# First tile's attention on f32 operands as loaded, head orders replanned, last sums sent from where their parts were

## The chip, the cores and the metric

The kernel runs on one core of a Trainium2 chip. A core has five engines that each work through their own list of instructions in order and meet at semaphores: TensorE (PE, matrix products into PSUM), VectorE (DVE), ScalarE (ACT), GpSimd (POOL) and SyncE (SP), which here issues every DMA. The metric is the device time of one execution in microseconds; lower is better.

## What is computed

Windowed attention over 32 heads, then two feed-forward blocks over 2304 tokens of width 512:

```python
batch, n_heads, seq, head_dim = (4, 8, 576, 64); window = 64
scores = (1/sqrt(D)) * q @ k.T
mask   = (rel >= 0) & (rel < window)          # rel = query position - key position
attn   = softmax(where(mask, scores, -1e9))
x      = attn @ v                             # then (B*S, H*D) = 2304 x 512
h      = max(x @ w1, x @ w2, x @ w3)          # 512 -> 768
y      = h @ moe_w_out                        # 768 -> 512
h2     = y @ w_in                             # 512 -> 2048
g      = where(h2 >= 1, h2, where(h2 <= -1, 0, (h2 + 1)**2 / 4))
out    = g @ w_out                            # 2048 -> 512
```

Everything is float32 at the input and the output.

## The kernel before

**High and low parts.** Most products are made in three passes on a reduced type (`F32R`). An operand `x` is split: `hi` is a copy into the reduced type, `lo` is `x - hi`. A product is then hi*lo + lo*hi + hi*hi. So every operand costs a copy (`hi`, mostly on ACT) and a subtraction (`lo`, on DVE or POOL). In `order` listings and the profile these copies and subtractions appear under the helper lines L649 (ACT), L875 (DVE) and L1084 (POOL).

**Tiles.** The 2304 tokens are nine tiles of 256, taken in six pieces `PIECES = (1, 1, 1, 2, 2, 2)`. For each tile, attention runs in four steps, one for each pair of heads; there are 36 steps, numbered `s`. The first piece is steps 0 to 3. A step is a chain: load `k`, `q`, `v`; split them (`k_hi`, `q_hi`, `v_hi`, `k_lo`, `q_lo`, `v_lo`); `score` on PE (L523, L525: one matmul of 256 columns and one of 128 for each of four blocks of keys); `mask` (L897) and `max` (L904) on DVE; `exp` (L676) and `safe` (L685) on ACT; `invert` (L911) on DVE; `norm` (L1119) on POOL; `probs`, a transpose on PE (L535); `p_hi` on ACT and `p_lo` on DVE; `values` on PE (L544, L546); `cross` on ACT (L695) and `x_sum` on DVE (L922), which add the two halves of the result; and `x_hi`, `x_lo`, the operands of layer 1.

**Zeros.** The two heads of a pair lie on different partitions, so `qT` holds each head's queries beside zeros. `zeros` on DVE (L942) writes eight blocks of 64x512 before anything else.

**Layer 1.** For each piece, 18 groups of 12 matmuls (L560) multiply `xT` with `w1`, `w2`, `w3` (six groups for each). `group` on ACT or DVE takes the result out of PSUM. The weights come in 12 pieces `w0` to `w11` of 128x768 and are split as well (`w_hi`, `w_lo`); the first six groups need pieces 0 to 3. Group 0 needs `x_lo` of steps 0 to 3.

**Order.** Nothing is scheduled when the kernel runs. For steps up to about the middle of the second piece, the table `FIRST` lists for each engine, word by word, what comes next. After it, `in_order` sorts the rest by planned positions: `SPREAD` and `LAG` say how far `score` and `probs` lie ahead of `values`, in units of a layer 1 group, and `AROUND` where each engine's part of a step lies. `Q_LO_ON_DVE` and `V_HI_ON_POOL` choose the engine of two kinds. An engine never skips an instruction that waits.

**After layer 1.** Layer 2 (L585) and then layers 3 and 4 (L612, L632) follow, PE bound. Layer 4's sums for 384 tokens stay in six PSUM banks over a unit of work; there are six units. The first two leave as partial sums to DRAM (`part_dram`), come back into `part_in` and are added by `block_out` on DVE (L1038): `o_sb[b % 3] = acc4[b] + part_in[b]`. `o_sb` has room for three of the six blocks, so the fourth block waits until the first has been sent: `dve.wait_ge(out_dma[b % QB], 16 * (2 * nth + b // QB))`. After the last block its DMA ends the program.

Of the kernel before, what the change touches and what calls it, by code (L numbers as in the profile page):

```python
# [97 lines left out]
def steps_of(n):  # L98
# [13 lines left out]
        k0 q0 mask0 v0 k1 q1 v1 k2 q2 k3 q3 v2 v3 w0 w1 w2 w3 k4 q4 w4 w5 w6 k5 q5 w7 v4 mask1 w8 k6 q6 w9  # L112
        w10 w11 v5 k7 q7 v6 k8 q8 v7 k9 q9 v8
    """,
    "PE": """
        score0 score1 score2 probs0 values0 score3 probs1 probs2 values1 values2 probs3 values3 score4
        score5 score6 group0 probs4 group1 group2 values4 group3 score7 group4 probs5 group5 group6
        values5 group7 group8 probs6 group9 group10
    """,
    "ACT": """  # L120
        k_hi0 q_hi0 v_hi0 k_hi1 q_hi1 v_hi1 k_hi2 q_hi2 exp0 safe0 k_hi3 q_hi3 exp1 safe1 p_hi0 w_hi0 exp2
        w_hi1 cross0 safe2 v_hi2 q_hi4 p_hi1 x_hi0 k_hi4 w_hi3 p_hi2 exp3 cross1 safe3 q_hi5 v_hi3 x_hi1
        k_hi5 w_hi4 cross2 p_hi3 w_hi7 x_hi2 cross3 q_hi6 k_hi6 exp4 x_hi3 safe4 w_hi11 v_hi5 k_hi7 q_hi7
# [4 lines left out]
        zeros0 zeros1 q_lo0 q_lo1 mask0 max0 q_lo2 invert0 mask1 max1 invert1 mask2 p_lo0 max2 w_lo1
        invert2 x_sum0 mask3 p_lo1 max3 w_lo3 p_lo2 x_sum1 invert3 x_sum2 p_lo3 w_lo7 mask4 x_sum3 max4
        q_lo6 mask5 invert4 max5 q_lo7 mask6 invert5 max6 p_lo4 w_lo5 w_lo9 invert6 w_lo4 w_lo6 x_sum4  # L130
        mask7 p_lo5 max7 group6 invert7 x_sum5 group7 w_lo10 group8 p_lo6 group9
# [1137 lines left out]
```

## Time and profile before

| | us |
|---|---|
| median of three runs | 804.43 (803.88 to 804.71) |
| the profiled execution, its own time | 805.22 |
| span of its trace, first to last instruction | 803.1 |
| PE busy in the span | 773.7 (96%) |
| DVE, ACT, POOL busy | 421.0, 406.5, 437.3 |

The span is what the views show; the execution's own time is 2.1 us longer. Times inside the trace are microseconds from the span's start. A matmul's duration includes its pipeline, so the distance between two starts is the better measure of what one costs. The page's second part gives PE's granted clock in 40 slices: with full speed as 1.0 it is 0.9 and 0.6 in the first two, 0.7 in the third and 1.0 after that apart from one slice at 0.9.

### The profile page before, as it was taken

The numbers are of one execution on the slowest core, as the hardware profiler recorded it, in microseconds if no ns is written. First come the engines' busy times: TensorE is split into PE (matmuls) and PEld (weight loads), VectorE is DVE, ScalarE is ACT, GpSimd is POOL, SyncE is SP. The second block draws the span as 40 slices with busy tenths as digits, with TensorE's granted clock in tenths as the row PEclk, the third lists the DMA queues.
The fourth block names the chain that finished last, engine by engine and source line by source line (L and its number), as shares of the span: only waits on it lengthen the run. The fifth ranks groups of instructions, "written<-read, shape, count | busy, mean of one in ns | idle before, by whom it ended". The sixth has DMA issues, their size and how long they took to land.

```text
span 803.1 us, 12567 instructions
## 1 busy us (share of the span) xinstructions
PE 773.7 (96%) x4320; PEld 704.7 (88%) x4320; DVE 421.0 (52%) x903; ACT 406.5 (51%) x957; POOL 437.3 (54%) x355
## 2 busy tenths in 40 slices
PE   4589999999999999999999999999999999999997
PEld 4589999988888888899997898899888999988996
DVE  6666476544644521227316573374777456357434
ACT  7865788657566322044525455355455446345331
POOL 6867779755666325025517475266666447248221
PEclk9679999999999999999999999999999999999999
DMA  7611322221220021002001102002111001200302
GB/s 233 222 57 57 110 70 81 96 69 55 80 72 27 27 80 52 1 8 98 0 0 52 53 1 79 1 2 80 53 52 53 1 1 61 98 1 27 131 1 79
DMA packets 25193, 46.56 MB, mean 58 GB/s; under 512 B 2352, under 2 KB 5552, under 8 KB 25136
## 3 DMA queue, kind: packets, MB, share of 16 engines
q1 hardware_dynamic: 25136, 45.82, 17.3%
q8 instruction: 33, 0.54, 0.3%
q14 instruction: 24, 0.20, 0.1%
HBM read 37.95 MB, written 7.86 MB: 57 GB/s over the span
## 4 chain that ended last, share of the span: by engine, by line
PE 90%; DVE 5%; ACT 3%; issue 1%; DMA 1%; SPq 0%; DVEq 0%; ACTq 0%
PE wide L560 28%; PE wide L632 22%; PE bank L612 21%; PE wide L585 9%; PE wide L544 3%; PE wide L523 3%; PE bank L535 2%; DVE g_sq L1026 2%; PE wide L546 1%; PE wide L525 1%; ACT g_sq L807 1%; ACT prob L676 1%; DMA v_nat<-v_dram 1%; DVE g L1031 0%; DVE prob L904 0%
## 5 line engine op out<-in xcount | busy, mean ns | idle before, releaser
L560 PE MATMUL wide<-xT,w 128*128 128x256 f32 (+1 forms) x1296 | 241.6, 342 | 0.0
L560 PEld LDWEIGHTS wide<-xT,w 128*128 128x128 f32 x1296 | 200.6, 191 | 23.7
L632 PE MATMUL wide<-w4s,gT 128*128 128x512 f32 x864 | 210.1, 392 | 0.0
L1084 POOL TENSOR_TENSOR gT<-g,gT 128x384 fp32r<-128x384 f32 x96 | 105.6, 1110 | 185.8 <-ACT gT L649 185.8
L612 PE MATMUL bank<-yT,w3s 128*128 128x384 f32 x1008 | 188.9, 337 | 3.1 <-issue 1.6
L632 PEld LDWEIGHTS wide<-w4s,gT 128*128 128x128 f32 x864 | 161.1, 188 | 31.2
L612 PEld LDWEIGHTS bank<-yT,w3s 128*128 128x128 f32 x1008 | 177.8, 188 | 11.2 <-DVE g L1031 4.0
L807 ACT ACTIVATE g_sq<-g_sq,half 128x384 f32<-128x384 f32 x96 | 58.1, 615 | 128.4 <-DVE g_sq L1026 128.1
L1014 DVE TENSOR_TENSOR pu<-bank,pu 128x384 f32<-128x384 f32 x72 | 40.1, 558 | 135.8 <-PE bank L612 129.0
L1031 DVE TENSOR_TENSOR g<-pu,g_sq 128x384 f32<-128x384 f32 x72 | 61.5, 854 | 36.2 <-ACT g_sq L807 35.6
L933 DVE TENSOR_TENSOR h<-wide,h 128x256 f32<-128x256 f32 (+1 forms) x72 | 40.1, 556 | 75.7 <-PE wide L560 75.3
L676 ACT ACTIVATE prob<-prob,neg_max 128x128 f32<-128x128 f32 x144 | 56.0, 391 | 41.9 <-DVE neg_max L904 41.6
L585 PE MATMUL wide<-h1s,wo 128*128 x432 | 75.3, 334 | 0.2 <-DVE h1s L875 0.2
L585 PEld LDWEIGHTS wide<-h1s,wo 128*128 128x128 f32 x432 | 74.9, 188 | 0.5 <-issue 0.5
L1119 POOL TENSOR_TENSOR prob<-prob,row_inv 128x512 f32<-128x512 f32 x36 | 38.1, 1060 | 57.3 <-DVE row_inv L911 57.1
L649 ACT ACTIVATE gT<-g 128x384 fp32r<-128x384 f32 x96 | 47.9, 521 | 41.0 <-DVE g L1031 40.9
L1084 POOL TENSOR_TENSOR v_part<-v_nat,v_part 128x512 fp32r<-128x512 f32 x36 | 47.6, 1322 | 17.9 <-ACT v_part L649 17.6
L1026 DVE TENSOR_SCALAR g_sq<-pu 128x384 f32<-128x384 f32 x72 | 54.0, 751 | 2.5
L523 PE MATMUL wide<-kT,qT 128*128 128x256 f32 x144 | 41.2, 362 | 13.9 <-DVE qT L875 8.5
L803 ACT ACTIVATE pu<-bank 128x384 f32<-128x384 f32 x72 | 34.4, 477 | 23.9 <-PE bank L612 23.9
L544 PE MATMUL wide<-pT,v_part 128*128 128x256 f32 x144 | 38.6, 345 | 7.6 <-DVE pT L875 3.8
L922 DVE TENSOR_TENSOR x_sums<-wide,o_cross 64x256 f32<-64x256 f32 x72 | 30.3, 420 | 29.5 <-ACT o_cross L695 28.4
(69 smaller groups left out, 963.4 us busy)
## 6 DMA issues: line engine op xcount, KB each, us to landing
v_nat<-v_dram SPq DMA_DIRECT2D x36, 256.0 KB, 2.7
raw<-w_dram SPq DMA_DIRECT2D x16, 512.0 KB, 3.5
h<-moe_w_dram SPq DMA_DIRECT2D x12, 384.0 KB, 6.1
out_dram<-o_sb SPq DMA_DIRECT2D x18, 256.0 KB, 2.1
k_in<-k_dram SPq DMA_DIRECT2D x12, 288.0 KB, 3.5
q_in<-q_dram SPq DMA_DIRECT2D x12, 256.0 KB, 2.9
part_dram<-o_sb SPq DMA_DIRECT2D x12, 256.0 KB, 2.1
part_in<-part_dram SPq DMA_DIRECT2D x2, 1536.0 KB, 7.3
```

Source lines behind the costliest of these rows:

```text
L523: pe.matmul(s_ps[:, b, :, :].rearrange("p x n -> p (x n)"), qT[:, n % 2, 0, j, :, :].rearrange("p h n -> p (h n)"), kT[:, n % 2, :, keys], ...
L544: pe.matmul(o_ps[:, b, :, :].rearrange("p x n -> p (x n)"), v_part[:, 0, s % 2, b, :], pT[:, :, s % 2, cols], start=True, stop=False, skip ...
L560: mm = pe.matmul(acc[gr % 2][:, 0:cols], w123[:, wp, w, kc, c * P:(c + 1) * P], xT[:, x_side(t), xp, kc, 0:cols], start=(kc == x == 0), st ...
L585: mm = pe.matmul(acc[c % 2][:, 0:MTOK], wo1[:, wp, kc, c * P:(c + 1) * P], h1s[:, of(t, 1), hp, kc, :].rearrange("p a n -> p (a n)"), star ...
L612: mm = pe.matmul(bank[:, 0:MTOK], w3s[j % HALF_F][:, wp, W_OF[m], kc * P:(kc + 1) * P], yT[:, m, yp, kc, :], start=(m in (0, 1, 3) and kc ...
L632: mm = pe.matmul(acc4[b], gT[:, k, gp, tb * P:(tb + 1) * P], w4s[pair_f(g) % HALF_F][:, wp, f, :], start=(first and x == 0), stop=(last an ...
L649: return act.activation(dst, src, ACT.Copy)
L676: act.activation(prob[:, s % 2, b, :], prob[:, s % 2, b, :], ACT.Exp, bias=neg_max[:, s % 2, b:b + 1], scale=-1.0, accum_out=row_sum[:, s ...
L807: act.activation(g_sq[:, k % 2, :], g_sq[:, k % 2, :], ACT.Square, bias=half[:, 0:1], scale=0.5).then_inc(squared, 1)
L1026: dve.tensor_scalar(g_sq[:, k % 2, :], output(g_at, k), -1.0, 1.0, ALU.max, ALU.min).then_inc(clamped, 1)
L1031: dve.tensor_tensor(g[:, k % 2, :], output(g_at, k), g_sq[:, k % 2, :], ALU.max).then_inc(g_done, 1)
L1084: return pool.tensor_tensor(dst, src, high.bitcast(F32), ALU.subtract)
```

## The change

**First piece plain.** Steps 0 to 3 no longer split `q`, `k`, `v` and the probabilities. `q`, `k` and `v` are loaded straight into their own f32 tiles (`q_plain`, `k_plain`, `v_plain`, one set for each pair), the score and values products are f32 matmuls of 128 columns, `max` reads the mask itself and there is no `mask` step, and the result goes from PSUM to `x_hi` (two halves on ACT) and `x_lo` (two halves, now on DVE) with no `cross` and no `x_sum`. `p_hi` of these steps is a plain copy, and has no `p_lo`. `q_plain` is loaded in two DMAs for each pair, in runs of 64 floats. The zeros of `qT`, which later pieces need, are written by two POOL memsets of 128x2048; DVE writes eight of 64x256 in `q_plain`.

**Orders.** `FIRST`, `SPREAD`, `LAG`, `AROUND`, `Q_LO_ON_DVE` and `V_HI_ON_POOL` have new contents.

**Last sums.** `block_out` on DVE writes its sum over `part_in[b]` instead of into `o_sb`, and SP sends it from there; the wait on `out_dma` is gone. The last block is added and sent in two halves. The reload of `part_in` now waits for the sends of the unit before it.

```diff
 def in_order(engine):
+            if i < PAIRS and (kind in SPLIT_KINDS or (engine, kind) == ("POOL", "x_lo")):
+                continue
...
-SPREAD = {1: (1.43, 2.27), 2: (2.24, 1.07), 3: (0, 2.0), 4: (0.6, 2.1), 5: (0, 1.9)}
-LAG = {1: (5.95, 1.63), 2: (5.04, 1.51), 3: (4.4, 2.1), 4: (5.0, 1.8), 5: (5.3, 1.8)}
+SPREAD = {1: (3.96, 1.1), 2: (3.63, 1.15), 3: (0.52, 1.88), 4: (2.16, 2.13), 5: (1.14, 2.82)}
+LAG = {1: (4.0, 1.44), 2: (4.45, 1.66), 3: (3.67, 1.4), 4: (4.26, 1.96), 5: (5.24, 1.92)}
...
         def k_in_of(n):
+            if a == 0:
+                sp.dma_start(k_plain[n][:, :], k_dram[:, u, start:start + cols]).then_inc(k_plain_in[n], 16)
+                return
...
         def q_in_of(n):
+            if a == 0:
+                for h in range(2):
+                    rows, _ = diagonal(h)
+                    sp.dma_start(q_plain[n][rows, :, h, :],
+                                 q_dram[rows, u, start:start + cols].rearrange("p (j n) -> p j n", n=BLK)).then_inc(q_plain_in[n], 16)
+                return
...
         def come_back(pair):
             for tb in range(QB):
-                sp.wait_ge(out_dma[tb], 16 * 2 * (pair + 1))
+                sp.wait_ge(out_dma[tb], 16 * 2 * (pair + 1 if pair == 1 else len(LEAVE) - 1))
...
+        def plain_score(s):
+            pe.wait_ge(off_diagonal, 2 * (s + 1))
+            pe.wait_ge(q_plain_in[s], 2 * 16)
+            pe.wait_ge(k_plain_in[s], 16)
+            after(pe, mask_added, NB * (scores_before(s) + 1))
+            for b in range(NB):
+                mm = pe.matmul(scores_of(s)[:, b, 0, :], q_plain[s][:, b, :, :].rearrange("p h n -> p (h n)"),
+                               k_plain[s][:, b * BLK:b * BLK + SPAN], start=True, stop=True, skip_group_check=True)
...
+        def plain_values(s):
+            pe.wait_ge(v_plain_in[s], 16)
+            pe.wait_ge(p_hi, s + 1)
+            after(pe, x_plain_lo, 2 * s)
+            for b in range(NB):
+                mm = pe.matmul(o_ps[:, b, 0, :], v_plain[:, s, b, :], p_plain[:, s % 2, b * P:(b + 1) * P],
+                               start=True, stop=True, skip_group_check=True)
...
+        def x_lo_of(s):
+            for h in range(2):
+                rows, cols = diagonal(h)
+                dve.wait_ge(x_plain_hi, 2 * s + h + 1)
+                lo(x_of(s, 1)[rows, :].rearrange("p (b n) -> p b n", b=NB), o_ps[rows, :, 0, cols],
+                   x_of(s, 0)[rows, :].rearrange("p (b n) -> p b n", b=NB)).then_inc(x_plain_lo, 1)
...
-            dve.wait_ge(out_dma[b % QB], 16 * (2 * nth + b // QB))
-            dve.tensor_tensor(o_sb[:, b % QB, :], acc4[b], part_in[:, b, :], ALU.add).then_inc(dve_out, 1)
+            cols = DM // 2 if unit == len(UNIT_PAIR) - 1 and b == BLOCKS - 1 else DM
+            for at in range(0, DM, cols):
+                dve.tensor_tensor(part_in[:, b, at:at + cols], acc4[b][:, at:at + cols], part_in[:, b, at:at + cols], ALU.add)\
+                    .then_inc(dve_out, 1)
...
+        for side in range(2):
+            pool.memset(qT[:, side, :, :, :, :].bitcast(F32), 0.0).then_inc(off_diagonal_parts, 1)
```

How the order moves, at three places. First ACT from its start; `prob` is the exponentials, `pT` and `p_plain` the turned probabilities, `w_50` the weights, `kT`, `qT`, `v_part` the split operands. Before:

```order
2 L649 ACTIVATE kT<-k_in 128x320
3 L649 ACTIVATE qT<-q_in 64x4x64 x2
4 L649 ACTIVATE v_part<-v_nat 128x512
5 L649 ACTIVATE kT<-k_in 128x320
6 L649 ACTIVATE qT<-q_in 64x4x64 x2
7 L649 ACTIVATE v_part<-v_nat 128x512
8 L649 ACTIVATE kT<-k_in 128x320
9 L649 ACTIVATE qT<-q_in 64x4x64 x2
10 L676 ACTIVATE prob,row_sum<-prob,neg_max 128x128 x4
```

And now:

```order
2 L738 ACTIVATE prob,row_sum<-prob,neg_max 128x128 x4
3 L747 ACTIVATE safe<-row_sum,tiny 128x4
4 L738 ACTIVATE prob,row_sum<-prob,neg_max 128x128 x4
5 L747 ACTIVATE safe<-row_sum,tiny 128x4
6 L709 ACTIVATE p_plain<-bank 128x512
7 L738 ACTIVATE prob,row_sum<-prob,neg_max 128x128 x4
8 L709 ACTIVATE w_50<-h_49 128x768
9 L747 ACTIVATE safe<-row_sum,tiny 128x4
10 L709 ACTIVATE xT<-wide 64x256 x2
```

The eight copies of `k`, `q` and `v` that stood ahead of the first exponentials are gone. The second place is PE just before layer 1's first group (L560 before, L616 now). Before, the last matmuls of the score of step 6 stand ahead of it, behind those of steps 4 and 5:

```order
90 L523 MATMUL wide<-kT,qT 128x256
91 L525 MATMUL wide<-kT,qT 128x128
92 L560 MATMUL wide<-xT,w_50 128x256 x12
93 L535 MATMUL bank<-ident,prob 128x128 x4
94 L560 MATMUL wide<-xT,w_50 128x256 x24
```

Now, from the transpose of step 2 on, with the score of step 4 ending at row 20 and that of step 5 beginning at row 22:

```order
9 L578 MATMUL bank<-ident,prob 128x128 x4
10 L586 MATMUL wide<-p_plain,v_plain 128x128 x4
11 L578 MATMUL bank<-ident,prob 128x128 x4
12 L586 MATMUL wide<-p_plain,v_plain 128x128 x4
...
20 L565 MATMUL wide<-kT,qT 128x128
21 L616 MATMUL wide<-xT,w_50 128x256 x36
22 L563 MATMUL wide<-kT,qT 128x256
```

One score (step 4) stands ahead of group 0 instead of three, and the scores of steps 5 and 6 stand behind groups 2 and 5. The third place is SP's first loads; `h_49` is where the weights arrive. Before:

```order
7 L436 DMA v_nat<-v_dram 128x512
8 L424 DMA k_in<-k_dram 128x320
9 L431 DMA q_in<-q_dram 128x256
10 L424 DMA k_in<-k_dram 128x320
11 L431 DMA q_in<-q_dram 128x256
12 L436 DMA v_nat<-v_dram 128x512 x2
13 L446 DMA h_49<-moe_w_dram 128x768 x4
```

And now:

```order
7 L440 DMA k_plain_66<-k_dram 128x320
8 L451 DMA q_plain_62<-q_dram 64x4x64 x2
9 L462 DMA v_plain<-v_dram 128x512
10 L440 DMA k_plain_67<-k_dram 128x320
11 L451 DMA q_plain_63<-q_dram 64x4x64 x2
12 L462 DMA v_plain<-v_dram 128x512 x2
13 L474 DMA h_49<-moe_w_dram 128x768 x8
```

None of the rows up to 13 waits for a buffer any more, each `q` is two DMAs, and eight pieces of weights follow in a row instead of four.

## Rows read from the trace of the kernel before

**Rows 1.** The chain of work that ended last, by engine (the page's fourth part)

```profile
PE 90%; DVE 5%; ACT 3%; issue 1%; DMA 1%; SPq 0%; DVEq 0%; ACTq 0%
```

**Rows 2.** Stretches: from:to, length, busy us of PE, PEld, DVE, ACT, POOL, PEclk, DMA

```profile
10.00:20.00 10.00, 6.97 (x31) 6.26 (x31) 6.02 (x32) 8.74 (x33) 8.23 (x9) 1.00 0.89 295
...
0.00:44.30 44.30, 23.17 (x104) 21.07 (x105) 29.63 (x92) 34.74 (x102) 32.21 (x40) 0.78 0.63 207
44.30:81.00 36.70, 36.70 (x295) 36.70 (x295) 24.49 (x67) 20.41 (x62) 25.02 (x24) 0.93 0.21 62
```

**Rows 3.** Timeline of PE: start, us, what xcount [idle before it <-releaser]

```profile
14.41 1.09 PE L535 MATMUL bank<-ident,prob 128*128 128x128 f32 x4
...
42.56 0.55 PE L523 MATMUL wide<-kT,qT 128*128 128x256 f32 x1 [2.06 <-DVE neg_max L904]
...
44.30 2.87 PE L560 MATMUL wide<-xT,w 128*128 128x256 f32 x12
...
47.67 3.73 PE L560 MATMUL wide<-xT,w 128*128 128x256 f32 x24
...
52.12 1.64 PE L560 MATMUL wide<-xT,w 128*128 128x256 f32 x12
53.59 0.28 PE L523 MATMUL wide<-kT,qT 128*128 128x256 f32 x1
...
54.47 1.65 PE L560 MATMUL wide<-xT,w 128*128 128x256 f32 x12
```

**Rows 4.** Timeline of ACT in the head

```profile
3.07 0.47 ACT L649 ACTIVATE kT<-k_in 128x320 fp32r<-128x320 f32 x1 [0.99 <-DMA k_in<-k_dram]
...
10.89 0.40 ACT L676 ACTIVATE prob<-prob,neg_max 128x128 f32<-128x128 f32 x1 [0.53 <-DVE neg_max L904]
...
13.20 0.84 ACT L649 ACTIVATE qT<-q_in 64x256 fp32r<-64x256 f32 x2
14.24 0.40 ACT L676 ACTIVATE prob<-prob,neg_max 128x128 f32<-128x128 f32 x1 [0.20 <-DVE neg_max L904]
...
15.92 0.30 ACT L685 ACTIVATE safe<-row_sum,tiny 128x4 f32<-128x4 f32 x1
...
16.64 0.84 ACT L649 ACTIVATE w<-h 128x768 fp32r<-128x768 f32 x1
```

**Rows 5.** Timeline of DVE in the head

```profile
10.56 0.29 DVE L904 CUSTOM_DVE_ANT_0 prob<-wide,prob 128x128 f32<-128x128 f32 x1 [0.19 <-DVE prob L897]
...
24.37 1.64 DVE L875 TENSOR_TENSOR w<-h,w 128x768 fp32r<-128x768 f32 x1
```

**Rows 6.** Timeline of POOL in the head

```profile
0.73 0.20 POOL L1130 MEMSET ident<- 128x128 f32 x1 [0.29 <-POOLq L1264]
...
13.23 1.04 POOL L1119 TENSOR_TENSOR prob<-prob,row_inv 128x512 f32<-128x512 f32 x1 [1.61 <-DVE row_inv L911]
...
17.65 1.83 POOL L1084 TENSOR_TENSOR w<-h,w 128x768 fp32r<-128x768 f32 x1
```

**Rows 7.** SP's timeline in the head

```profile
1.65 0.42 SPq L442 DMA_DIRECT2D mask<-masks_dram  x1
```

**Rows 8.** DMA issues of the first 60 us: count, size, median us to landing

```profile
q_in<-q_dram SPq DMA_DIRECT2D x10, 128.0 KB, 3.1
mask<-masks_dram SPq DMA_DIRECT2D x1, 256.0 KB, 4.0
```

**Rows 9.** Timeline around step 8: the last score matmul and the normalization

```profile
78.97 0.22 PE L525 MATMUL wide<-kT,qT 128*128 128x128 f32 x1
...
83.20 1.04 POOL L1119 TENSOR_TENSOR prob<-prob,row_inv 128x512 f32<-128x512 f32 x1 [2.11 <-DVE row_inv L911]
```

**Rows 10.** Timeline of the program's end, all engines

```profile
790.53 8.36 PE L632 MATMUL wide<-w4s,gT 128*128 128x512 f32 x36
...
795.59 2.05 DVE L1038 TENSOR_TENSOR o_sb<-wide,part_in 128x512 f32<-128x512 f32 x3 [3.06 <-PE wide L632]
...
798.50 2.02 DVE L1038 TENSOR_TENSOR o_sb<-wide,part_in 128x512 f32<-128x512 f32 x3 [0.86 <-DMA out_dram<-o_sb]
```

More of the change, by code:

```diff
@@ L118 @@
-        values5 group7 group8 probs6 group9 group10
+        score0 score1 score2 probs0 values0 probs1 score3 values1 probs2 values2 probs3 values3 score4
+        group0 group1 group2 score5 group3 group4 probs4 group5 score6 group6 values4 group7 probs5 score7
+        group8 group9 values5 probs6 group10
     """,
     "ACT": """
-        k_hi0 q_hi0 v_hi0 k_hi1 q_hi1 v_hi1 k_hi2 q_hi2 exp0 safe0 k_hi3 q_hi3 exp1 safe1 p_hi0 w_hi0 exp2
-        w_hi1 cross0 safe2 v_hi2 q_hi4 p_hi1 x_hi0 k_hi4 w_hi3 p_hi2 exp3 cross1 safe3 q_hi5 v_hi3 x_hi1
@@ L123 @@
-        k_hi5 w_hi4 cross2 p_hi3 w_hi7 x_hi2 cross3 q_hi6 k_hi6 exp4 x_hi3 safe4 w_hi11 v_hi5 k_hi7 q_hi7
-        exp5 w_hi9 safe5 p_hi4 group0 exp6 group1 safe6 group2 cross4 v_hi6 w_hi10 group3 k_hi8 group4
-        p_hi5 x_hi4 group5 exp7 safe7 cross5 v_hi7 x_hi5 k_hi9 p_hi6 q_hi8 q_hi9
+        exp0 safe0 exp1 safe1 p_hi0 exp2 w_hi0 safe2 x_hi0 p_hi1 w_hi2 w_hi3 exp3 x_hi1 safe3 p_hi2 w_hi4
+        w_hi7 k_hi4 q_hi4 x_hi2 p_hi3 q_hi5 k_hi5 w_hi9 x_hi3 w_hi10 exp4 group0 safe4 v_hi4 q_hi6 group1
@@ L126 @@
+        k_hi6 group2 k_hi7 q_hi7 w_hi6 group3 v_hi5 group4 p_hi4 exp5 group5 safe5 exp6 cross4 safe6 v_hi6
+        p_hi5 x_hi4 exp7 cross5
     """,
     "DVE": """
[L128 to L131, printed above, removed]
+        zeros0 zeros1 zeros2 zeros3 max0 max1 invert0 invert1 max2 w_lo1 invert2 x_lo0 max3 w_lo3 x_lo1
@@ L132 @@
+        invert3 w_lo7 x_lo2 w_lo5 mask4 x_lo3 max4 w_lo10 invert4 q_lo6 mask5 q_lo7 max5 p_lo4 mask6
+        invert5 max6 group6 w_lo8 invert6 group7 p_lo5 x_sum4 mask7 group8 max7 group9 w_lo11
     """,
     "POOL": """
-        k_lo0 v_lo0 k_lo1 v_lo1 k_lo2 norm0 k_lo3 norm1 w_lo0 w_hi2 norm2 v_lo2 x_lo0 k_lo4 norm3 x_lo1
-        v_lo3 k_lo5 x_lo2 v_hi4 w_lo2 k_lo6 x_lo3 norm4 v_lo4 k_lo7 w_hi5 norm5 w_hi6 norm6 v_lo5 x_lo4
-        v_lo6 w_hi8 norm7 w_lo8 w_lo11
+        norm0 norm1 w_hi1 w_lo0 norm2 w_lo2 norm3 w_hi5 k_lo4 w_lo4 k_lo5 v_lo4 norm4 k_lo6 w_lo6 k_lo7
@@ L137 @@
+        w_hi8 norm5 w_hi11 v_lo5 norm6 w_lo9 x_lo4
     """,
@@ L532, in probs @@
             pe.wait_ge(normed, s + 1)
-            after(pe, p_lo, s - 1)
+            if s < 2 + PAIRS:
+                after(pe, p_hi, s - 1)
+            else:
+                pe.wait_ge(p_lo, s - 1 - PAIRS)
             for b in range(NB):
@@ L565, in _ @@
         for kind, i in in_order("PE"):
-            if kind == "score":
+            if kind == "score" and i < PAIRS:
+                plain_score(i)
+            elif kind == "values" and i < PAIRS:
+                plain_values(i)
+            elif kind == "score":
                 score(i)
@@ L938, in _ @@
             if kind == "zeros":
[L939 to L942 removed]
+                for h in range(2):
+                    rows, _ = diagonal(h)
+                    dve.memset(q_plain[i][rows, :, 1 - h, :], 0.0).then_inc(off_diagonal, 1)
             elif kind == "q_lo":
@@ L954, in _ @@
                 x_sum_of(i)
+            elif kind == "x_lo":
+                x_lo_of(i)
             elif kind == "w_lo":
```

176 lines of the change are left out of this document (104 added, 72 removed).

## The prediction

> **What bounds the kernel now.** I read the chain of waits first: PE carries 90% of it [rows 1]. Nearly all matmuls are untouched by the change, so time can only come from where PE isn't working, from PE's half rate, or from the tail. The windows show where PE isn't working: up to 44.30, where layer 1 begins, PE is busy for 23.17 of 44.30 us; in the 36.70 us after that it never stops [rows 2]. The reader is to see that from 44.30 on the time is a row of matmuls, and that before it ACT is the fullest engine (34.74 us, against 32.21 on POOL and 29.63 on DVE). So the main question is at what time group 0 of layer 1 begins, and the second is what is left for PE then. The last stretch is the end: PE's final matmuls run from 790.53 to 798.89, but DVE's last three sums begin only at 798.50, after 0.86 us of waiting for the send of the first, and end at 800.52; the program ends at 803.1 [rows 10].
>
> **When group 0 begins, worked forward.** Prices first. A score or values step at PE's half rate takes 44.30 - 42.56 = 1.74 us, at full rate 54.47 - 53.59 = 0.88 [rows 3]. Four exponentials take 15.92 - 14.24 = 1.68, `safe` and `p_hi` together 16.64 - 15.92 = 0.72, a weight's `hi` 0.84, `k_hi` 0.47, a two-half copy of 64x256 0.84 [rows 4]; this last is also my price of the new `x_hi`. `norm` is 1.04 [rows 6]. The first exponential follows its `max` by 10.89 - 10.56 = 0.33 [rows 4, 5].
>
> An f32 matmul of 128 columns on real data isn't in the trace. The nearest below are the f32 transposes: four in 1.09 us with the pipeline, so about 0.2 each at half rate, 0.8 a step [rows 3]. Above I take four such turns for each matmul: 0.8 each, 3.2 a step. I take 0.44 each, 1.76 a step, hence the same as the two matmuls it replaces. That rests on four streams of 128 columns at what 128 columns of the 256-column matmuls cost at half rate (12 of them in 47.67 - 44.30 = 3.37 less the 0.7 of four transposes between, 0.22 each, 0.11 for 128 columns). The Trainium skill (FP8 and Floating Point Precision, "TensorE Precision Notes") says true FP32 takes four passes through the array, which is the same count; no row here shows whether each pass also reloads its weights, and that is a rival below.
>
> The walk, with ends of work: `k0` landed by 3.07 [rows 4]. `q0` is now two DMAs, the second issued where the mask's was, at 1.65, and with 3.1 to landing it is there at 4.8; the mask goes out one place (0.47) later and with 4.0 to landing arrives at 6.1 [rows 7, 8]. Score 0 runs 4.8 to 6.5, the first exponential starts at 7.0 instead of 10.89. Then ACT is the thread: `exp0`, `safe0`, `exp1`, `safe1` to 10.8; `norm0` ends at 10.6, its transpose at 11.6, `p_hi0` at 12.2, values 0 at 14.0; meanwhile ACT does `exp2`, `w_hi0`, `safe2`, and `x_hi0` at 15.8; DVE's `x_lo0` at 16.8 lets values 1 run to 18.7. `p_hi1`, two weights, `exp3` (19.7), `x_hi1`, `safe3`, `p_hi2` at 21.3; values 2 to 23.1; two weights, `k_hi4`, `q_hi4`, `x_hi2`, `p_hi3` at 25.7; values 3 to 27.5, the score of step 4 to 29.3. `x_lo3`, which only the last quarter of group 0 needs, is at about 31, in time. ACT's own work to `x_hi3` is 4 x 2.40 + 6 x 0.84 + 4 x 0.84 + 2 x 1.31 = 20.6 us, from 7.0 to 28.7 with 1.1 us idle: ACT is nearly solid, so the walk can't be beaten by much. I add 0.7 us for subtractions that stretch when DVE and POOL work together (a weight's `lo` takes 1.64 on DVE and 1.83 on POOL [rows 5, 6]). **Group 0 at 30.0 instead of 44.3: -14.3 us**, bounds 28.5 and 33 with this price of an f32 step.
>
> Two costs are hidden. The two POOL memsets of 128x2048 hold sixteen times the elements of the 128x128 one of 0.20 us [rows 6], so at most 3.2 us each; from 1.5 they end by 7.9, before `norm0` starts at 9.6. Without that cover each further us would delay `norm0` by one. Weight pieces: SP has 17 DMAs ahead of `w0` and issues one each 0.47 us, so `w0` goes out at 8.7. Ahead of and with `w0` and `w1` there are 3.2 MB; at the 295 GB/s of the stretch 10 to 20 [rows 2] that is 10.8 us and a first landing at about 3.1, so `w1` is there near 14. POOL's `w_hi1`, which `norm2` stands behind, ends at 15; DVE's `w_lo1`, which `invert2` and `x_lo0` stand behind, at 16. That is within 0.2 us of the walk, so there is no cover to spare here.
>
> **What moves behind group 0.** The scores of steps 5 and 6 were done before 44.30 and now follow groups 2 and 5: 2 x 0.88 = **+1.8 us**. For the other engines, ACT gets about 7 us more to do between groups 0 and 18 (`exp4`, `exp5`, the copies of `q`, `k`, `v`), DVE 5, POOL 3. They were busy 20.4, 24.5 and 25.0 us of 36.7 there [rows 2], so 27 to 30 of about 38 now: they fit. But each queue is in order, and pieces such as `w_lo6` come, in the same kind of walk, only 1.5 us ahead of the group that needs them. I allow **+0.8 us** of new PE waits, bounds 0 and 4.
>
> **Half rate.** At 44.30 the granted clock is at its lower level (1.2 GHz); PE has worked without a break since 42.56, and of the 24 matmuls from 47.67 most still go slowly (3.73 us with pipeline, where 12 take 53.59 - 52.12 = 1.47 at 2.4 GHz) [rows 3]. Group 0 and the transposes behind it thus lose 3.37 - 1.47 - 0.35 = 1.55 us (the transposes at half of 0.7), and the two groups from 47.67, with 0.17 taken off for the pipeline (1.64 - 1.47), 3.56 - 2.94 = 0.62: 2.2 us. After the change PE works without a break from 25.8, 4.2 us ahead of group 0 instead of 1.7, so I expect 1.4 us lost: **-0.8**, bounds -1.5 and +1.
>
> **Later pieces of layer 1.** The replan changes which work stands beside which, not how much. From the end of a score to the end of its `norm` it took 84.24 - 79.2 = 5.0 us at step 8 [rows 9]. By the orders, priced by the rows above, there were 9 to 14 us between a score and its transposes from step 8 on; now there are 6.8 to 11.4. Still more than 5.0: nothing, with -0.5 to +2 kept inside the bounds above.
>
> **Tail.** PE finishes a block each 0.69 us (three matmuls); DVE's sums take 0.69 and follow from 795.59 [rows 10]. With no wait, block 3 starts at 797.65, block 5 at 799.03, its first half ends near 799.4 and its second near 799.85, against 800.52. The last send is half as long. From the last sum to the end it was 803.1 - 800.52 = 2.6; I take 2.5. **-0.8**, bounds -0.5 and -1.2. The reload of `part_in` waits some 2 us longer but is needed a whole unit later.
>
> **Sum.** -14.3 + 1.8 + 0.8 - 0.8 - 0.8 = -13.3. The profiled execution took 805.22, so the new one 791.9; it lay 0.8 above the median of 804.43, so the median is **791.1**. The forecast's own range is 787 to 795.
>
> **Rivals.** *The f32 step is dear* (3.2 us at half rate). Then PE is the thread of the head: 8 x 3.2 + 4 transposes x 0.8 + 1.74 = 30.5 us from 4.8, plus about 1.7 us waiting for the first softmax and for `p_hi`: group 0 at 37, 7 us later, 798. For: at half rate a transpose of 128 columns costs 0.2, twice what 128 columns of a wider matmul cost, so something beside the stream sets it and could be paid in each pass. Against: nothing in the trace. If it is as cheap as a transpose, group 0 starts near 28.5, because ACT doesn't go faster, 789.6.
>
> *The loads are late.* If the many short runs hold the queues at the 207 GB/s of the whole head [rows 2], 3.2 MB take 15.5 us and `w1` comes at 18.6, 4.6 us later, and `x_lo0`, values 1 and all behind them slide nearly as much: 795.5. The Trainium skill (DMA: Bandwidth & Descriptors, "Specifications") gives 512 bytes as the smallest transfer at line rate, and the new `q` runs have 256; it speaks against this change, and would by itself double the time of half a megabyte, some 1.5 us. No row has such runs.
>
> *The tighter replan starves PE: slower.* If with shorter leads the chain from score to transpose in pieces 2 to 5 (28 steps) takes longer than the order leaves, PE waits at each step. 0.48 us a step eats the 13.3 us; at 0.8 a step it costs 28 x 0.8 = 22.4 us, and the time is 791.1 + 22.4 = 813.5. For: the lead fell from 11.4 to 7.8 in the fourth piece. Against: 5.0 measured, and PE runs without a pause at such spacing.
>
> *The head isn't bound by the split* but by something that stays, such as the weights; then only the tail counts: 803.6. Against it: ACT is busy 34.74 of 44.30 us, some 10 of them with copies that go away.
>
> **How the numbers follow.** Chances: forecast 0.69; dear f32 step 0.14; late loads 0.10; starved replan 0.04; head unchanged 0.03. Below 787 and above 799 there is little but the last two and the forecast's edges, so the range is 786.5 to 798.5. A measurement of this kernel tells 0.2% (1.6 us) from no change: faster 0.93, same 0.03, slower 0.04.
>
> **What would show it.** Right: the first exponential near 7.0, group 0 at 29 to 31, ACT hardly idle before it, f32 matmuls 0.4 to 0.5 apart, DVE's last six sums without a gap. Wrong: f32 matmuls 0.8 apart with PE solid from 5 us; ACT or POOL waiting for `h`; gaps ahead of L578 or L598 in layer 1; waits of PE on `w_lo` pieces 4 to 11.

## The result

The changed kernel takes **825.39 us** (median of 6 runs, 824.25 to 826.02), the kernel before 804.45 (6 runs): ratio 1.0259, 95% interval 1.0247 to 1.0272. It is 21 us slower, where 13 us faster was forecast. The profiled execution took 824.25, with a span of 822.5.

The head does what was forecast. PE in the changed kernel, from the first score to group 0 of layer 1 (start, us, engine, line, what, xcount, [idle before it <-releaser]; a plain step is four f32 matmuls, each two instructions here):

```profile
5.08 2.05 PE L548 MATMUL wide<-k_plain,q_plain 128*128 128x128 f32 x8 [5.08 <-DMA q_plain<-q_dram]
...
13.73 2.05 PE L586 MATMUL wide<-p_plain,v_plain 128*128 128x128 f32 x8 [0.78 <-ACT p_plain L709]
15.57 1.06 PE L578 MATMUL bank<-ident,prob 128*128 128x128 f32 x4
...
24.48 2.05 PE L586 MATMUL wide<-p_plain,v_plain 128*128 128x128 f32 x8 [1.07 <-DVE xT L943]
...
28.41 1.13 PE L586 MATMUL wide<-p_plain,v_plain 128*128 128x128 f32 x8 [1.02 <-ACT p_plain L709]
...
31.07 1.29 PE L616 MATMUL wide<-xT,w 128*128 128x256 f32 x9
32.91 2.05 PE L616 MATMUL wide<-xT,w 128*128 128x256 f32 x15 [0.55 <-DVE xT L943]
```

Group 0 begins at 31.07 instead of 44.30 [rows 3], and an f32 step costs 15.57 - 13.73 = 1.84 us. The views give a granted clock of 1.00 there; that this step ran at half rate (1.2 GHz) is read from its duration, the same 2.05 us as at 24.48, where they give 0.50, against 1.13 us at 28.41, where they give 1.00. The reader then has to look at the stretches behind it. These are the changed kernel's, cut (here to whole microseconds) where layer 1 passes from one piece to the next, with the last two pieces in one row (from:to, length, busy us of PE, PEld, DVE, ACT, POOL, granted clock, DMA):

```profile
31.00:70.00 39.00, 36.49 (x302) 35.65 (x301) 27.94 (x77) 25.00 (x76) 27.06 (x27) 1.00 0.30 90
70.00:116.00 46.00, 40.39 (x327) 39.67 (x326) 26.82 (x99) 27.00 (x86) 26.99 (x26) 0.96 0.21 68
116.00:170.00 54.00, 46.14 (x357) 45.53 (x356) 26.72 (x96) 34.78 (x107) 35.12 (x34) 0.91 0.21 69
170.00:250.00 80.00, 72.68 (x389) 62.30 (x388) 37.90 (x129) 45.24 (x136) 40.09 (x37) 0.96 0.17 55
250.00:363.00 113.00, 113.00 (x565) 95.79 (x564) 39.66 (x108) 37.45 (x100) 40.16 (x28) 1.00 0.13 43
```

and these the kernel before's, cut at the same work:

```profile
44.30:80.50 36.20, 36.20 (x290) 36.20 (x290) 24.02 (x62) 20.28 (x61) 24.52 (x24) 0.93 0.21 63
80.50:121.00 40.50, 39.93 (x341) 39.76 (x340) 24.55 (x98) 31.55 (x101) 29.90 (x30) 1.00 0.29 89
121.00:162.00 41.00, 40.76 (x347) 40.46 (x345) 26.09 (x95) 30.15 (x95) 34.39 (x33) 1.00 0.29 88
162.00:230.60 68.60, 68.60 (x388) 59.59 (x387) 36.05 (x125) 41.97 (x129) 40.66 (x38) 1.00 0.21 68
230.60:343.00 112.40, 112.40 (x559) 95.03 (x559) 36.35 (x98) 36.40 (x93) 43.84 (x31) 1.00 0.12 41
```

From group 0 to the end of layer 1 it now takes 332.0 us, before 298.7: 33.3 more, over the second, third and fourth stretch above all. PE is idle 23.3 us of it (332.0 - 308.7), before 0.8, so 22.5 more. By my estimate from the clock column, half rate behind the pauses takes about 10 us (4% of 46, 9% of 54 and 4% of 80) where it took 2.5 before (7% of 36.2), and the two scores that moved take 1.8; some 1.6 us of the 33.3 stay unexplained. No engine is full: POOL is busy 169.4 of 332.0 us. So PE waits for engines that are themselves half idle. For whom it waits, over the whole span (engine, line, what it waited for: us in total, times, longest):

```profile
PE bank L578 <- POOL prob L1205: 11.2, 6, 5.8
PE wide L616 <- DVE h L1014: 6.8, 4, 3.1
...
PE wide L616 <- POOL xT L1168: 4.0, 1, 4.0
```

and for whom POOL waits, in the changed kernel from 31 to 330:

```profile
POOL xT L1168 <- ACT xT L709: 77.0, 25, 7.8
POOL prob L1205 <- DVE row_inv L985: 26.2, 14, 3.9
POOL kT L1168 <- ACT kT L709: 11.3, 6, 3.7
```

The same view of the kernel before, in the same window:

```profile
POOL prob L1119 <- DVE row_inv L911: 53.6, 20, 6.9
POOL xT L1084 <- ACT xT L649: 17.4, 10, 5.6
...
POOL kT L1084 <- ACT kT L649: 0.8, 3, 0.3
```

Before, POOL stood mostly at `norm`, the next thing PE needed. Now it stands at `x_lo` (written `xT`), which PE doesn't need before the next piece, with the operands and the `norm` of other steps behind it. The longest pause shows it. First POOL, then PE:

```profile
216.07 0.73 POOL L1168 TENSOR_TENSOR xT<-x_sums,xT 128x256 fp32r<-128x256 f32 x1 [6.73 <-ACT xT L709]
216.76 1.27 POOL L1168 TENSOR_TENSOR v_part<-v_nat,v_part 128x512 fp32r<-128x512 f32 x1
217.99 1.40 POOL L1168 TENSOR_TENSOR kT<-k_in,kT 128x576 fp32r<-128x576 f32 x1
219.35 2.59 POOL L1168 TENSOR_TENSOR qT<-q_in,qT 64x512 fp32r<-64x512 f32 x2
222.02 1.04 POOL L1205 TENSOR_TENSOR prob<-prob,row_inv 128x512 f32<-128x512 f32 x1
```

```profile
223.11 1.11 PE L578 MATMUL bank<-ident,prob 128*128 128x128 f32 x4 [5.78 <-POOL prob L1205]
```

ACT's `x_hi`, for which POOL stood 6.73 us, ran at 215.59, behind exponentials, a `v_hi` and a `q_hi`; the reciprocal that the normalization at 222.02 needs was there at 215.90 (DVE, 215.72 and 0.18 long). Six microseconds passed while POOL worked off what the plan had put ahead of it. Not all of the pause is the standing at `x_lo`: the `v_lo`, `k_lo` and `q_lo` ahead of `norm` take 5.3 us by themselves, and two of them had their operands only when ACT's `v_hi` and `q_hi` were done, at 214.19 and 215.36.

POOL isn't the only one that stands. The second longest wait of the table, `PE wide L616 <- DVE h L1014`, goes through ACT and DVE. Its longest pause is the 3.12 us ahead of 106.80. First ACT, then DVE:

```profile
102.30 0.69 ACT L709 ACTIVATE kT<-k_in 128x576 fp32r<-128x576 f32 x1 [2.69 <-PE wide L565]
```

```profile
104.81 0.88 DVE L1003 TENSOR_TENSOR x_sums<-wide,o_cross 64x256 f32<-64x256 f32 x2 [4.97 <-ACT o_cross L757]
...
106.33 0.41 DVE L1014 TENSOR_TENSOR h<-wide,h 128x256 f32<-128x256 f32 x1
```

ACT stood at an early `k_hi`, whose buffer an older score still used. `cross` ran behind it at 104.19, DVE stood 4.97 us at `x_sum` for `cross`, and the copy that empties the PSUM bank of layer 1 (DVE's `h`) came behind that.

The tail, DVE's last sums in the changed kernel, to be held against [rows 10]:

```profile
815.72 4.15 DVE L1121 TENSOR_TENSOR part_in<-wide,part_in 128x512 f32<-128x512 f32 x7 [3.07 <-PE wide L692]
```

One piece of 4.15 us from 815.72 to 819.87, where before it was 4.93 with a gap.

### The profile page after: what moved, and what is told of

It is laid out like the page before. It is cut to its first block, busy times and chain, and to the rows that moved or that the text cites. A ratio compares the mean times of both kernels' runs of the same rounds, so it can differ in the third digit from the quotient of the medians.

```text
span 822.5 us, 12502 instructions
## 1 busy us (share of the span) xinstructions
PE 780.4 (95%) x4320; PEld 708.5 (86%) x4320; DVE 419.5 (51%) x897; ACT 401.8 (49%) x943; POOL 419.0 (51%) x334
## 4 chain that ended last, share of the span: by engine, by line
PE 76%; ACT 6%; POOL 6%; DVE 6%; issue 4%; DMA 2%; SPq 0%; DVEq 0%; ACTq 0%; POOLq 0%
PE wide L692 22%; PE bank L672 20%; PE wide L616 19%; PE wide L645 8%; PE wide L598 2%; DVE g_sq L1108 2%; ACT prob L738 2%; PE bank L578 2%; POOL prob L1205 1%; DMA q_in<-q_dram 1%; POOL v_part L1168 1%; PE wide L563 1%; ACT qT L709 1%; POOL kT L1168 1%; PE wide L548 1%
## 5 line engine op out<-in xcount | busy, mean ns | idle before, releaser
L616 PE MATMUL wide<-xT,w 128*128 128x256 f32 (+1 forms) x1296 | 245.1, 345 | 12.0 <-DVE h L1014 6.8
L616 PEld LDWEIGHTS wide<-xT,w 128*128 128x128 f32 x1296 | 204.5, 194 | 38.1 <-DVE h L1014 7.5
L1113 DVE TENSOR_TENSOR g<-pu,g_sq 128x384 f32<-128x384 f32 x72 | 61.4, 853 | 36.2 <-ACT g_sq L875 35.6
L1014 DVE TENSOR_TENSOR h<-wide,h 128x256 f32<-128x256 f32 (+1 forms) x72 | 39.7, 553 | 67.2 <-PE wide L616 66.5
L1168 POOL TENSOR_TENSOR xT<-x_sums,xT 128x256 fp32r<-128x256 f32 x32 | 23.5, 735 | 77.1 <-ACT xT L709 77.0
L1003 DVE TENSOR_TENSOR x_sums<-wide,o_cross 64x256 f32<-64x256 f32 x64 | 27.0, 422 | 49.4 <-ACT o_cross L757 46.2
L1168 POOL TENSOR_TENSOR v_part<-v_nat,v_part 128x512 fp32r<-128x512 f32 x32 | 42.2, 1318 | 7.0 <-ACT v_part L709 4.9
L1168 POOL TENSOR_TENSOR yT<-t_sums,yT 128x768 fp32r<-128x768 f32 x20 | 39.4, 1979 | 7.1 <-ACT yT L709 7.1
```

Source lines behind the costliest of these rows:

```text
L616: mm = pe.matmul(acc[gr % 2][:, 0:cols], w123[:, wp, w, kc, c * P:(c + 1) * P], xT[:, x_side(t), xp, kc, 0:cols], start=(kc == x == 0), st ...
L1113: dve.tensor_tensor(g[:, k % 2, :], output(g_at, k), g_sq[:, k % 2, :], ALU.max).then_inc(g_done, 1)
L1168: return pool.tensor_tensor(dst, src, high.bitcast(F32), ALU.subtract)
```

## The experiments

### Which table costs

**e1_oldplan** puts back all tables that plan the work behind the head's lists (except that `v_hi` of step 4, on POOL before, stays on ACT as the new head has it):

```diff
-SPREAD = {1: (3.96, 1.1), 2: (3.63, 1.15), ...
+SPREAD = {1: (1.43, 2.27), 2: (2.24, 1.07), ...
 (LAG, AROUND and Q_LO_ON_DVE as before, too)
-V_HI_ON_POOL = (1, 3, 8, 9, 12, 13, 15)
+V_HI_ON_POOL = (9, 13, 16, 21, 24, 32)
```

> The changed kernel with the plan tables of before (SPREAD, LAG, AROUND, and the engines of q_lo and v_hi, except that v_hi of step 4 stays on ACT); the head's lists are the new ones. If the new plan behind the head is what costs (33 us more between group 0 and the end of layer 1), the gain of the head comes through: 790 to 797. If instead the new head hands over too little work done ahead, whatever the plan, it stays at 815 or more.

Measured: 795.66 us, ratio to before 0.9896 (0.9881 to 0.9911), the only one of the first four kernels (e1 to e4) that has the whole new head and nothing of the new plan. The gain of the head comes through. Its stretches, cut at the same work:

```profile
31.70:71.10 39.40, 36.68 (x306) 36.07 (x306) 29.02 (x88) 27.65 (x87) 29.30 (x30) 1.00 0.28 82
71.10:111.70 40.60, 40.04 (x343) 39.87 (x341) 24.23 (x96) 31.76 (x101) 30.07 (x30) 1.00 0.29 89
111.70:152.70 41.00, 40.76 (x347) 40.45 (x345) 26.01 (x95) 30.05 (x95) 34.35 (x33) 1.00 0.30 90
```

From the second on they are as long as before, to 0.1 us. So behind the new head the new plan costs 825.39 - 795.66 = 29.7 us. Whether it would cost as much behind the old head was not run.

**e2_sp_only** and **e3_lag_only** put back one table each:

```diff
# e2_sp_only
-    "SP": {"k": ("score", -5.0), "q": ("score", -4.9), "v": ("values", -5.0)},
+    "SP": {"k": ("score", -4.5), "q": ("score", -4.6), "v": ("values", -4.0)},
# e3_lag_only: SPREAD and LAG as before
```

> The changed kernel with only SP's row of AROUND as before (k -4.5, q -4.6, v -4.0 instead of -5.0, -4.9, -5.0). If the loads of v that stand among those of k and q and wait for a buffer are the cause, most of the loss goes: 805 or less. If the shorter leads between score and values are the cause, it stays within 4 us of 825.

> The changed kernel with only SPREAD and LAG as before. If the shorter leads are the cause, 790 to 800. If SP's order is the cause, 810 or more, since it keeps its row.

Measured: 823.11 (1.0236, 1.0216 to 1.0256) and 837.69 (1.0422, 1.0402 to 1.0441). My first two theories fell: the loads' place carries 2 us at most (the intervals of the two ratios overlap), and with the long leads back but the new rows of `AROUND` it is 12 us slower still. That leaves the rows. (e3's time lies where the expectation put the case that SP's order is the cause; e2 rules that cause out.)

**e5_pool_row**, **e6_act_dve_rows** and **e7_xlo_only** put back rows of `AROUND` in the changed kernel, **e8_before_xlo** puts one new number into the kernel before:

```diff
# e5_pool_row
-    "POOL": {"k_lo": ("score", -3.0), "norm": ("score", 1.4), "v_hi": ("values", -1.4), "v_lo": ("values", -1.2),
-             "x_lo": ("values", 0.7)},
+    "POOL": {"k_lo": ("score", -0.7), "norm": ("score", 2.0), "v_hi": ("values", -1.9),
+             "v_lo": ("values", -0.9), "x_lo": ("values", 1.55)},
# e6_act_dve_rows: the rows of ACT and DVE as before
# e7_xlo_only
-             "x_lo": ("values", 0.7)},
+             "x_lo": ("values", 1.55)},
# e8_before_xlo, in the kernel before
-             "v_lo": ("values", -0.9), "x_lo": ("values", 1.55)},
+             "v_lo": ("values", -0.9), "x_lo": ("values", 0.7)},
```

> The changed kernel with only POOL's row of AROUND as before. Theory X: the new row puts POOL's x_lo at 0.7 behind values, ahead of ACT's x_hi at 0.75, and its k_lo and norm early, so POOL stands and everything behind it comes late: 795 to 806. Rival Y, the rows of ACT and DVE (p_hi at 0.2, x_sum at 0.45) are the cause: stays above 815.

> The changed kernel with only the rows of ACT and DVE as before. Theory X: POOL goes on standing, 815 or more. Rival Y: 795 to 806.

> The changed kernel with one number changed back: POOL's x_lo at 1.55 behind values instead of 0.7. Theory X, if x_lo is the whole of it: 797 to 808. If it is one part of several in POOL's row: 808 to 818. Rival Y: within 3 us of 825.

> The kernel before with one number of the change: POOL's x_lo at 0.7 instead of 1.55. Theory X: POOL waits at x_lo with norm behind it, 810 to 825. Rival Y: within 3 us of 804.

Measured: 814.29 (1.0124, 1.0104 to 1.0143), 877.89 (1.0913, 1.0894 to 1.0931), 825.93 (1.0260, 1.0243 to 1.0277) and 850.17 (1.0566, 1.0548 to 1.0584). One number in the table of the kernel before costs 45 us; the same number put back in the changed kernel brings nothing. Against what was expected: e5 lies between the two theories, e6 goes with theory X and against Y, e7 lies where Y put it and outside both of X's ranges, and e8 goes with X in direction but is 25 us above its range. Neither theory had all four; Y falls by e6 and e8, and X falls in so far as it made `x_lo` in POOL's row the cause by itself. The rows belong together: POOL's waits from 31 to 330 show what each mixture makes of them. For e6_act_dve_rows:

```profile
POOL kT L1169 <- ACT kT L710: 86.0, 15, 10.9
POOL xT L1169 <- ACT xT L710: 54.3, 11, 7.3
```

For e7_xlo_only:

```profile
POOL prob L1205 <- DVE row_inv L985: 46.6, 19, 5.0
POOL v_part L1168 <- ACT v_part L709: 43.1, 16, 5.3
POOL kT L1168 <- ACT kT L709: 18.8, 7, 5.3
```

and what PE waits for there:

```profile
PE wide L616 <- POOL xT L1168: 6.9, 1, 6.9
...
PE wide L598 <- DVE x_sums L1003: 5.4, 1, 5.4
```

For e8_before_xlo, POOL and then PE:

```profile
POOL xT L1084 <- ACT xT L649: 116.2, 28, 8.9
POOL prob L1119 <- DVE row_inv L911: 7.4, 5, 2.3
```

```profile
PE wide L523 <- POOL qT L1084: 16.7, 8, 3.9
PE bank L535 <- POOL prob L1119: 8.9, 7, 2.6
```

In e6 POOL has `k_lo` at -3.0 and ACT its `k_hi` at -2.05: POOL is ordered to stand at each `k_lo`. In e7 POOL stands only 10.9 us at `x_lo`, but longer at `norm`, `v_lo` and `k_lo`. And a late `x_lo` isn't free there: PE waits 6.9 us for it at the start of a piece, and 5.4 us for an `x_sum`, which in the kernel's code may only overwrite `x_sums` when POOL's `x_lo` of the step before has read it. These two make 12.3 of the 23.3 us that PE is idle in e7's layer 1. In e8 POOL stands at `x_lo` 28 times, and what PE then misses most is `q_lo`, an operand of a score, and only after it `norm`. (The profiled execution of e8 took 844.89, 5 us less than its median.)

### Early places one at a time, on the good plan

The next four start from e1_oldplan (795.66), so that one thing is new in each:

```diff
# e9_newlag_oldrows: the new SPREAD and LAG
# e10_inputs_early
-"k_hi": ("score", -2.05)   "q_lo": ("score", -1.2)   "k_lo": ("score", -0.7)
+"k_hi": ("score", -3.5)    "q_lo": ("score", -3.0)   "k_lo": ("score", -3.0)
# e11_outputs_early
-"x_sum": ("values", 0.75)   "x_lo": ("values", 1.55)
+"x_sum": ("values", 0.45)   "x_lo": ("values", 0.7)
# e12_softmax_early
-"max": 0.45  "invert": 1.45  "norm": 2.0   "p_hi": 0.35  "p_lo": 0.75
+"max": 0.6   "invert": 1.3   "norm": 1.4   "p_hi": 0.2   "p_lo": 0.6
```

> The kernel e1_oldplan with only the new SPREAD and LAG. Theory Z, the rows of AROUND are what costs and the leads themselves are harmless: 793 to 800. If the shorter leads cost by themselves: above 805.

> The kernel e1_oldplan with the splits of k and q planned early as in the change (k_hi at -3.5, q_lo and k_lo at -3.0 from the score; the loads where they were). If an engine that stands at an operand which is not there yet is what costs, PE loses here: 805 to 825. If only the results' side costs: within 3 us of 796.

> The kernel e1_oldplan with x_sum at 0.45 and x_lo at 0.7 from values, as in the change. Theory Z: POOL stands at x_lo as in e8 (119 us there), 810 to 840, a part of it saved against e8 because x_sum comes earlier too. If x_lo is harmless once x_sum is early: within 4 us of 796.

> The kernel e1_oldplan with the middle of a step as in the change: max 0.6, invert 1.3, norm 1.4, p_hi 0.2, p_lo 0.6. Theory Z: POOL stands at norm instead of elsewhere, and ACT at p_hi: 800 to 815. If only the two ends of a step cost: within 3 us of 796.

Measured: 803.32 (0.9988, 0.9978 to 0.9997), 815.13 (1.0129, 1.0112 to 1.0146), 838.37 (1.0422, 1.0399 to 1.0445) and 817.88 (1.0164, 1.0147 to 1.0181). e10 and e11 lie in the ranges of the theory that standing costs; e9 lies between its two ranges and e12 is 3 us above its upper one. Each group of early places costs alone, 19.5, 42.7 and 22.2 us, and the shorter leads 7.7. The whole new plan costs 29.7, less than the dearest alone, so the effects don't add. A likely reason, not tested, is that where softmax is early too, POOL's `norm` is ahead of the `x_lo` that it would have stood behind. The new places of `v_hi` and `v_lo` were never run alone. POOL's waits in e12_softmax_early name its own place to stand:

```profile
POOL prob L1206 <- DVE row_inv L986: 88.1, 27, 6.7
```

### How the cost grows, and the other side

```diff
# on e1_oldplan
# e13_xlo_mid:  x_lo 1.55 -> 1.15
# e14_xlo_late: x_lo 1.55 -> 2.2
# e15_new_sets: the new Q_LO_ON_DVE and V_HI_ON_POOL
# on e9_newlag_oldrows
# e16_newlag_xlo_late: x_lo 1.55 -> 2.0
```

> The kernel e1_oldplan with POOL's x_lo at 1.15 instead of 1.55 (e11 has 0.7, with x_sum earlier). If POOL's standing at x_lo is what costs, it grows with the distance: POOL stands 40 to 90 us at x_lo and the time is 800 to 820. If there is an edge at x_hi's own place (0.75) that decides, 1.15 costs nothing: within 3 us of 796.

> The kernel e1_oldplan with x_lo at 2.2. If only standing costs: within 3 us of 796, since nothing waits for x_lo until the next piece, and POOL stands less than 14 us there. If every place but the tuned one costs: above 800.

> The kernel e1_oldplan with the new choice of engines (Q_LO_ON_DVE, V_HI_ON_POOL). Work moved between engines that are 50 to 60% busy: within 4 us of 796. If the sets carry a part of the 30 us: above 800.

> The kernel e9_newlag_oldrows (803.3) with x_lo at 2.0 instead of 1.55. With the new leads POOL stood 55 us at x_lo. If that standing is how the leads cost: 795 to 800. If the lead itself is too short for the chain: within 2 us of 803.

Measured: 805.84 (1.0014, 1.0002 to 1.0026), 796.44 (0.9901, 0.9884 to 0.9917), 800.51 (0.9956, 0.9942 to 0.9970) and 806.36 (1.0024, 1.0014 to 1.0033). POOL's and PE's waits in e13_xlo_mid, from 31 to 330:

```profile
POOL xT L1169 <- ACT xT L710: 82.5, 23, 7.0
POOL prob L1206 <- DVE row_inv L986: 10.3, 6, 2.6
```

```profile
PE wide L564 <- POOL qT L1169: 4.3, 3, 1.8
```

In the same window POOL's waits in e1_oldplan are

```profile
POOL prob L1206 <- DVE row_inv L986: 50.2, 18, 6.9
POOL v_part L1169 <- ACT v_part L710: 15.0, 6, 5.7
POOL xT L1169 <- ACT xT L710: 14.0, 7, 5.7
```

In e11_outputs_early they are 116.9 us at `x_lo` and 4.8 at `norm`. This is a scale for `x_lo`: at 1.55, 1.15 and 0.7 POOL stands at it 14.0, 82.5 and 116.9 us, and the time is 795.7, 805.8 and 838.4 (e11 has `x_sum` earlier as well, and e8 without that, on the other head, also 116.2). The first 68 us of standing cost 10, the next 34 cost 33. The waits say why the first part is cheap: most of it isn't new. POOL's waits at `norm` and `v_lo` went away meanwhile, 65.2 us in e1 and 10.3 in e13, so that the three together are 79.2, 92.8 and 121.7 us: 14 more, then 29 more. POOL's place in `AROUND` behind ACT's `x_hi` (0.75) is no protection either, since at 1.15 it still stood 82.5 us.

Late costs 0.8 us (e14), which the runs can't tell from nothing. So it is early places that cost, not any change of place. The engine choices carry 4.9 us on this plan (e15), where I had expected at most 4. And the new leads don't cost through POOL's standing at `x_lo`: later by 0.45 it is 3 us slower, not faster (e16), outside both ranges; that theory fell. Its trace has the other side of `x_lo` instead: DVE's `x_sum` waits 6.9 us for the `x_lo` of the step before it (4.9 in e9), and PE's values 5.2 us for `x_sum` (3.1 in e9).

### The leads, piece by piece

**e17_lag1_new** takes from the new leads only those of the second piece:

```diff
# on e1_oldplan
-SPREAD = {1: (1.43, 2.27), ...   LAG = {1: (5.95, 1.63), ...
+SPREAD = {1: (3.96, 1.1), ...    LAG = {1: (4.0, 1.44), ...
```

> The kernel e1_oldplan with the new leads for the second piece alone (SPREAD[1], LAG[1]). In e9 the stretch from group 0 to group 18 took 36.8 us against 39.4 in e1, and the two after it 4.6 and 6.0 more. If each piece's leads act in their own stretch: 793 to 794, better than both kernels of the case. If the hand-over to the next piece is what costs in e9: 797 or more.

Measured: **793.77 us** (793.23 to 794.0), ratio to before 0.9868 (0.9851 to 0.9884): better than both kernels of the case. It is 1.9 us less than e1_oldplan, as was expected. The shorter lead of the second piece pays beside the new head: from group 0 at 32.7 to group 18 at 70.0 it takes 37.3 us, where e1_oldplan took 39.4. Why it does was not tested; the engines have more to do there (DVE 29.0 us of the 39.4, before 24.0 of 36.2). The cost of the new leads lies in the pieces behind.

### The tail alone

**e4_tail_only** is the kernel before with the new last sums, the sends and the reload of `part_in` that go with them:

```diff
...
-            dve.wait_ge(out_dma[b % QB], 16 * (2 * nth + b // QB))
-            dve.tensor_tensor(o_sb[:, b % QB, :], acc4[b], part_in[:, b, :], ALU.add).then_inc(dve_out, 1)
+            cols = DM // 2 if unit == len(UNIT_PAIR) - 1 and b == BLOCKS - 1 else DM
+            for at in range(0, DM, cols):
+                dve.tensor_tensor(part_in[:, b, at:at + cols], acc4[b][:, at:at + cols], part_in[:, b, at:at + cols], ALU.add)\
+                    .then_inc(dve_out, 1)
...
```

> The kernel before with only the change of the last sums (added over part_in and sent from there, the last block in halves). Sum of the prediction: 0.8 us less than before (0.5 to 1.2), 803.6; no gap among the last sums. The rival: the send bounds the end, nothing is gained.

Measured: 803.88 against 804.30, ratio 0.9994 (0.9985 to 1.0003): no difference that the runs can tell. In its trace the gap is gone:

```profile
790.10 8.36 PE L636 MATMUL wide<-w4s,gT 128*128 128x512 f32 x36
...
795.17 4.16 DVE L1043 TENSOR_TENSOR part_in<-wide,part_in 128x512 f32<-128x512 f32 x7 [3.07 <-PE wide L636]
```

and from PE's last matmuls (790.10) to the end of the span (801.9) it takes 11.8 us, before 803.1 - 790.53 = 12.6. The 0.8 us is there in one execution of each; the medians show 0.4, inside their noise.

## Why the prediction was wrong

**The head was right in the main.** First exponential at 7.61 (forecast 7.0), group 0 at 31.07 (forecast 30.0, bounds 28.5 and 33), an f32 step 1.84 us at half rate (taken as 1.76, bounds 0.8 and 3.2). The Trainium skill (FP8 and Floating Point Precision, "TensorE Precision Notes") says that true FP32 takes four passes. The 0.46 us of one f32 matmul agrees with four streams at the 0.11 us that the prediction took for each; the trace shows two instructions for each matmul and no passes, so it can't confirm the count. The first memsets on POOL took 3.54 us together and ended at 4.95, hidden as said. What the walk had too early was `w1`: POOL's copy of it waited for the load until 16.34 instead of 14, and `x_lo0` with values 1 came later. The queues moved 169 and 338 GB/s in the first two stretches of 10 us; the runs don't separate what the 256-byte pieces of `q` took of that, so the 512 bytes that the Trainium skill gives as the smallest transfer at line rate (DMA: Bandwidth & Descriptors, "Specifications") were not tested. That runs of 256 bytes would double the time was my estimate, and it stays open.

**The sum was right for the change without its plan.** e1_oldplan has group 0 at 31.7 (-12.6 against -14.3 in the sum), +3.2 us to group 18 (+1.8 for the two scores, +0.8 for new waits and -0.8 for half rate forecast, thus 1.8), and nothing behind it. Its span is 10.2 us shorter, the forecast -13.3: the term for group 0 was 1.7 too good, and the terms behind it 1.4. Part of that nearness is luck: up to group 18 PE was idle 39.40 - 36.68 = 2.7 us where I had allowed 0.8, and half rate gave back about 2.5 us (0.07 of 36.2 before, nothing in e1) where I had put 0.8. The two errors cancel in good part.

**The step that failed is "Later pieces of layer 1".** I said that the replan changes which work stands beside which, not how much, and set it at nothing, with -0.5 to +2. It cost 29.7 us. Two things were wrong in it. I measured the chain from the end of a score to the end of its normalization at one step, as 5.0 us [rows 9]. Counted along the trace that is step 9 and not 8, and it is the shortest of all from 8 to 27: by the same measure the median of these twenty is 6.9 us and the longest 9.0. Against the 6.8 to 11.4 us that I had worked out for the new order, "still more than 5.0" would have read as no cover to spare. And I compared this with the distance on PE's order alone. That order holds what PE waits for, but whether the other engines deliver in time is set by their own order: the rows of `AROUND`. The front part of the document quotes `SPREAD` and `LAG` and not those rows, and the prediction didn't weigh them. Much of it could be read without a run: POOL's `x_lo` at 0.7 stands ahead of ACT's `x_hi` at 0.75, which it needs, and `k_lo` at -3.0 half a unit behind a `k_hi` that itself waits until the buffer of two loads before is free.

**The rival on the slower side** (a starved replan, chance 0.04) had the direction and a part of the place: PE's waits at the transposes are 11.2 of its 23.3 idle us, and gaps ahead of L578 were named as a sign of being wrong. But it, too, made the cause the shorter leads. By e9 the leads cost 7.7 us alone, and by e3 putting them back in the changed kernel doesn't help. The rest comes with the rows, and there the traces show engines standing at operands that aren't there yet. The chance was far too low because the forecast read the plan of four engines off the order of one.

**The tail** was forecast at -0.8 and is -0.7 to -0.8 in the traces, unproven by the medians. **Half rate** came out on the other side of the sum: group 0 already ran at 2.4 GHz, but the granted clock fell to 1.2 GHz four times in layer 1, beside PE's four longest pauses there (3.12 us ahead of 106.80, 3.97 ahead of 121.29, 2.84 ahead of 150.06 and 5.78 ahead of 223.11). Beside the shorter ones, up to 2.07 us ahead of 96.84, it stayed at 2.4 GHz. After the one of 5.78 us a matmul of 256 columns and one of 128 took 0.43 to 0.46 us from start to start, where at 216.47 they took 0.23.

What stays open: why e15's engine choices cost 4.9 us, how the 29.7 us divide among the rows, what the places of `v_hi` and `v_lo` carry, and how the leads of the pieces behind the second share their 10 us (803.32 - 793.77). The interplay of the rows was shown only by its sums, with the waits of single traces beside them.

## What to carry to other kernels

When a change replaces an order, hold each engine's list against the others', not only the list of the engine that bounds: for each entry ask whether its operand is made at an earlier place in the maker's list, and what stands behind it if not. An engine that is half idle in total can still cost dearly, because what it waits for is decided by order. Read the sum of its waits and their names together: the wait at one name can rise while another falls (`x_lo` 68 us up and `norm` 40 us down from e1 to e13), so a single line can't be turned into a cost; and the sum rises by itself when the stretch gets longer, so it can't be called the cause either. What tells is the chain: for whom does the bounding engine wait, and at what did that engine stand before. Work that nobody needs soon goes late (here `x_lo`: late cost 0.8 us, early up to 45), but only as late as the next writer of its operand's buffer allows, as e7 and e16 show. And read a chain's latency from many steps, not from the first one that is easy to follow.

## What the runs showed of the hardware

An f32 matmul of 128 columns costs 1.84 / 4 = 0.46 us at half rate, where the pair of reduced-type matmuls that it replaces costs 0.43 (from 42.91 to 43.34 in the kernel before), and the profile shows it as two instructions. At 2.4 GHz the eight instructions of such a step took 1.13 us together, at 1.2 GHz 2.05. Two memsets of 128x2048 f32 on POOL took 3.54 us.
